# A chunked delta-rule attention on one core: products over the whole TensorE array in place of two 64x64 halves, and the step loop written out

## What is computed

```python
k_n = k / (np.linalg.norm(k, axis=-1, keepdims=True) + 1e-06)
state = np.zeros((B, H, D, D))
for t in range(S):
    y[:, :, t] = q[:, :, t] @ state
    v_old = k_n[:, :, t] @ state
    state = state + beta[:, :, t] * outer(k_n[:, :, t], v - v_old)
...
x = moe(x=y)          # 8 experts, each row goes to one
return moe2(x=x)      # three products, their maximum, one product
```

## Time and profile before

| what | value |
|---|---|
| median of 3 runs | 1251.17 us (1241.86 to 1251.54) |
| profiled execution | 1252.97 us, its span 1251.3 us |
| attention, from 0 to about 550 us | see the rows below |
| routing and sorting | 550 to 605 us |
| first expert layer | 605 to 923 us |
| second expert layer | 923 to 1251 us |
| instructions fetched over the span | 122 packets, 2.00 MB |

### The profile page before, as it was taken

The page is one execution under the profiler, slowest core; times in us unless marked ns, Lnnn a source line. Parts: engine busy times, 40 slices in busy tenths (PEclk is TensorE's granted clock), DMA queues, the critical chain, the costliest instruction groups (busy, mean ns, idle before and its releaser), DMA issues. The chain is left out here.

```text
span 1251.3 us, 38030 instructions
## 1 busy us (share of the span) xinstructions
PE 1025.1 (82%) x16548; PEld 907.0 (72%) x16549; DVE 477.0 (38%) x890; ACT 326.4 (26%) x636; POOL 338.1 (27%) x226
## 2 busy tenths in 40 slices
PE   2688888868868888850598889899959999999999
PEld 2677777767767877740487778787848888888888
DVE  1345454544435454442233343333324232232311
ACT  0334333434323343310121221212212121221211
POOL 3332233223403321118505544415531010000000
PEclk9989998989979899875799999999979999999999
DMA  8501111110111110005323423333320101100000
GB/s 295 217 19 50 36 32 36 48 37 19 50 35 35 33 33 18 3 3 193 119 103 132 138 78 108 127 128 113 113 60 29 32 20 44 31 25 26 1 26 26
DMA packets 34455, 83.51 MB, mean 67 GB/s; under 512 B 4240, under 2 KB 23184, under 8 KB 31760
## 3 DMA queue, kind: packets, MB, share of 16 engines
q1 hardware_dynamic: 28656, 45.22, 11.0%
q0 software_dynamic: 5664, 36.18, 8.7%
HBM read 58.58 MB, written 22.81 MB: 65 GB/s over the span
## 5 line engine op out<-in xcount | busy, mean ns | idle before, releaser
L1011 PE MATMUL hb<-early,last_h 128*128 128x512 f32 x648 | 204.8, 398 | 4.7 <-ACT o_sb L1125 3.6
L1011 PEld LDWEIGHTS hb<-early,last_h 128*128 128x128 f32 x648 | 121.1, 190 | 31.0 <-ACT o_sb L1125 2.7
L1011 PE MATMUL hb<-early,last_l 128*128 128x512 f32 x324 | 127.5, 393 | 0.0
L299 PEld LDWEIGHTS bank<-t,n_hi 64*64 64x64 f16 x2688 | 75.8, 114 | 22.3 <-issue 11.4
L299 PE MATMUL bank<-t,n_hi 64*64 64x64 f16 x2688 | 79.1, 198 | 11.5 <-issue 10.4
L456 ACT CAST t<-bank 128x512 f16<-128x512 f32 x96 | 56.3, 587 | 119.4 <-PE bank L299 117.8
L497 DVE TENSOR_TENSOR p<-bank,cf 128x512 f16<-128x512 f32 x96 | 66.0, 688 | 42.8 <-PE bank L299 41.9
L587 POOL COPY x_all<-y_tile 128x384 f32<-128x384 f32 (+1 forms) x24 | 12.5, 521 | 257.0 <-DVE y_tile L513 257.0
L933 POOL TENSOR_TENSOR late<-w_raw,late 128x3072 fp32r<-128x3072 f32 x8 | 59.7, 7457 | 71.5 <-DVE late L920 71.4
L1149 DVE TENSOR_TENSOR m<-hb,m 128x512 f32<-128x512 f32 x36 | 24.9, 692 | 132.8 <-PE hb L1011 132.8
L1011 PE MATMUL ob<-wo_h,early 128*128 128x384 f32 x288 | 74.2, 335 | 0.0
(11 more groups left out here) (154 smaller groups left out, 2271.6 us busy)
## 6 DMA issues: line engine op xcount, KB each, us to landing
w_raw<-w POOLq DMA_DIRECT2D x14, 1536.0 KB, 7.2
k_raw<-kh SPq DMA_DIRECT2D x24, 256.0 KB, 4.9
kq_t<-qh SPq DMA_DIRECT2D x24, 256.0 KB, 2.8
x_sorted<-zeros SPq DMA_DIRECT2D x32, 192.0 KB, 2.2
x_in<-x_sorted SPq DMA_DIRECT2D x29, 192.0 KB, 2.4
y_sorted<-y_sb SPq DMA_DIRECT2D x28, 192.0 KB, 1.9
v_in<-vh SPq DMA_DIRECT2D x24, 192.0 KB, 2.8
out<-o_sb SPq DMA_DIRECT2D x24, 192.0 KB, 1.9
```

The source lines that it names most:

```text
L299: ins = pe.matmul(out[s, C * u:C * u + C], lhs(s, u), rhs(s, u), start=first and u == 0, stop=True, skip_group_check=True)
L1011: ins = pe.matmul(out, a[x], b[y], start=first and i == 0, stop=last and i == 2, skip_group_check=True)
```

## The change

- **No loops.** `run` writes out all steps on every engine; indices are plain numbers.
- **n_hi block-diagonal.** `n_hi` gets twice the columns, head 0's block and head 1's block on the diagonal and zeros (set once) beside them. The new helper `both_heads` multiplies it in one product over 128 rows and 128 columns in place of two 64x64 ones: in jacobi, prod and resid. `whole` does so for `diagonal`. gram, turn, update, inv and the product with `n_lo` stay as they are.
- **kt from full transposes.** Four 128x128 transposes in place of sixteen 64x64 products.
- **The chain over the whole array.** `state`, `rhs` and `z` get the form [128, pair, 2 heads, 48], zero off the diagonal. "ks" multiplies keys and queries with the state at once (96 columns), "z" is 128 rows to 64 columns, "up" multiplies K' and A with z at once and adds to what "ks" left in the bank. A product of 8 columns precedes it.
- **K' from an own copy of the keys.** Four loads of k for each step rather than two (`k_own`, two buffers), and `kb` is made from it with a factor `beta_k` that DVE works out (NORM part 9).
- **Other engines.** DVE: rhs and the addition to the state in two instructions of 64 partitions each; the copy of y moves to ACT; the reset of the state is a memset at the end of a batch. ACT: n_hi and z in two instructions each, y in one. POOL: n_lo in two. SP: `k_own` loads stand between k and q in the queue, q lands in pieces of 64 numbers.

```diff
-        for w in range(-1, 4):
-            walk_of(w)
-        with eng.Fori(2, STEPS // 2 - 1) as m:
-            body(step(m, 0), step(m - 1, 1), step(m - 1, 0), step(m, 1))
-            body(step(m, 1), step(m, 0), step(m - 1, 1), step(m + 1, 0))
-        for w in range(STEPS - 2, STEPS + 2):
-            walk_of(w)
+        for w in range(-1, STEPS + 2):
+            body(*(k if 0 <= k < STEPS else None for k in (w, w - 1, w - 2, w + 1)))
...
+        def both_heads(lhs, rhs, out, first=False):
+            for u in range(U):
+                ins = pe.matmul(out[:, C * u:C * u + C], lhs[:, u].rearrange("q h c -> q (h c)"), rhs(u), start=first and u == 0,
+                                stop=True, skip_group_check=True)
+            return ins
+        def whole(lhs, rhs, out, first):
+            return pe.matmul(out[:, :], lhs, rhs, start=first, stop=True, skip_group_check=True)
...
-                for u in range(U):
-                    for s in half:
-                        ins = pe.matmul(tb[s, C * u:C * u + C], kn[par][st][s, u, :], ident[s, s], start=u == 0, stop=True,
+                for p in range(NP):
+                    ins = pe.transpose(tb[:, P * p:P * p + P], kn[par][st][:, 2 * p:2 * p + 2, :].rearrange("q h d -> q (h d)"), ident)
...
-                diagonal(ident16, ident_rep, pb, True)
-                each_head(n, eye if lv == 0 else t, pb).then_inc(jacobi_done[st], 1)
+                whole(ident16, ident_rep, pb, True)
+                both_heads(n, lambda u: ident_rep[:, 0:C] if lv == 0 else t16[st][:, u, :], pb).then_inc(jacobi_done[st], 1)
...
-                    for s, r in zip(half, rows):
-                        ins = pe.matmul(out[s, W + D * p:W + D * p + D], kq[r, 0, NP * e + p, :], state[st][r, p, :],
+                    ins = pe.matmul(out[:, W * p:W * p + W], kq_t[par][st][:, NP * e + p, :, :].rearrange("q a t -> q (a t)"),
+                                    state[st][:, p].rearrange("q h d -> q (h d)"), start=p == 0, stop=True, skip_group_check=True)
...
+                pe.matmul(out[0:C, X:X + 8], ident16[:, 0:C], ident16[:, 0:8], start=True, stop=True, skip_group_check=True)
                 for p in range(NP):
-                    for s, r in zip(half, rows):
-                        pe.matmul(out[s, D * p:D * p + D], kq[r, 1, NP * e + p, :], state[st][r, p, :], start=p == 0, stop=False,
...
+                    ins = pe.matmul(out[:, W * p:W * p + W], n_kb_a[par][st][:, NP * e + p, 1:3, :].rearrange("q a t -> q (a t)"),
+                                    z[st][:, p].rearrange("q h d -> q (h d)"), start=False, stop=True, skip_group_check=True)
...
-                act.copy(n_hi[st][:], n_p[par][st][:, :, 0, :]).then_inc(n_hi_ready[st], 1)
+                for hh, s in enumerate(half):
+                    act.copy(n_hi[st][s, :, hh, :], n_kb_a[par][st][s, :, 0, :]).then_inc(n_hi_ready[st], 1)
...
+            elif what == "up":
+                act.wait_ge(up_done[st], 2 * k + e + 1)
+                if e == 0 and k >= 1:
+                    act.wait_ge(x_out[st], k)
+                act.copy(y_tile[st][half[e], :], yb[st][C:P, 0:X]).then_inc(y_out[st], 1)
...
+            for st in range(2):
+                if k >= 2:
+                    sp.wait_ge(kb_ready[st], k - 1)
+                sp.dma_start(k_own[par][st][:], kh[2 * k + st]).then_inc(k_own_in[par], 16)
```

More of the change, by code:

```diff
@@ L39 @@
 CF_BASE = CF_LV + (LEVELS - 2) * C
[L40 to L41 removed]
+CF_TRI = CF_BASE + C
 CF_ONE = CF_TRI + P
@@ L282, in _ @@
             sp.dma_start(raw[:], w[0]).then_inc(arrived, 16)
[L283 to L291, removed]
+        load_k(2, 0)
+        for k in range(2, STEPS):
+            if k + 1 < STEPS:
+                load_k(k + 1, (k + 1) % 2)
+            load_qv(k, k % 2)
     @block.tensor
@@ L313, in eye, with inv @@
             return ident_rep[s, 0:C]
-        def inv(k, m, par, st, what, lv):
+        def inv(k, par, st, what, lv):
             tb, ttb, pb = bank[st]
-            n, nl, t, tt, pr = (lambda s, u, x=x[st]: x[s, u, :] for x in (n_hi, n_lo, t16, tt16, p16))
+            n = n_hi[st]
+            nl, t, tt, pr = (lambda s, u, x=x[st]: x[s, u, :] for x in (n_lo, t16, tt16, p16))
             if what == "kt":
@@ L356, in inv @@
                     pe.sem_inc(passed_pe, 1)
-                each_head(n, t, pb, first=True).then_inc(prod_done[st], 1)
+                both_heads(n, lambda u: t16[st][:, u, :], pb, first=True).then_inc(prod_done[st], 1)
             elif what == "update":
@@ L544, in norm @@
                 dve.wait_ge(s, 6 * k + 6)
-                if not before(k, 1):
+                if k >= 1:
                     for st in range(2):
@@ L548, in norm @@
                 dve.reciprocal(inverse, kept).then_inc(inv_norm, 1)
+            elif part == 9:
+                dve.wait_ge(inv_norm, k + 1)
+                if k >= 2:
+                    for st in range(2):
+                        dve.wait_ge(kb_ready[st], k - 1)
+                own = inverse.rearrange("q (s p h) -> q h s p", s=2, h=2)
+                b = beta[:, 1, 2 * k:2 * k + 2, :].rearrange("q s (p h) -> q h s p", h=2)
+                to = beta_k[par][:].rearrange("q s (e p) -> q e s p", e=2)
+                for e in range(2):
+                    for hh in range(2):
+                        ins = dve.tensor_tensor(to[half[hh], e], own[half[e], hh], b[half[e], hh], ALU.mult)
+                ins.then_inc(beta_k_ready, 1)
@@ L553, in _, with inv @@
+        dve.wait_ge(blank, 1)
         dve.wait_ge(const_in, 64)
-        run(dve, lambda a, c, b, n: walk(a, c, b, n, inv, chain, norm))
+        run(lambda a, c, b, n: walk(a, c, b, n, inv, chain, norm))
     @block.gpsimd
     def _(pool):
-        def inv(k, m, par, st, what, lv):
-            b = beta[:, 2 * k + st, :]
+        latest = [blank, 1]
+        def inv(k, par, st, what, lv):
+            b = beta[:, 0, 2 * k + st, :]
             if what == "kn":
                 pool.wait_ge(inv_norm, k + 1)
-                if not before(k, 2):
+                if k >= 2:
@@ L575, in inv @@
[L575 removed]
+                pool.wait_ge(n_hi_ready[st], 2 * k + 2)
+                pool.wait_ge(*latest)
+                for hh, s in enumerate(half):
+                    if hh == 1:
+                        pool.wait_ge(n_lo_ready[st], 2 * k + 1)
+                    pool.tensor_tensor(n_lo[st][s], n_kb_a[par][st][s, :, 0, :], n_hi[st][s, :, hh, :],
+                                       ALU.subtract).then_inc(n_lo_ready[st], 1)
```

248 lines of the change are left out of this document (121 added, 127 removed).

## The result

The changed kernel took 1206.43 us (median of 4 runs, 1203.6 to 1209.83), the kernel before 1246.86 us in the same job: a ratio of 0.968, 95% interval 0.962 to 0.974. It is faster, by 3.2%, where the forecast said 1.5% of this median (1228). The profiled execution took 1208.53 us with a span of 1206.9, against 1252.97 and 1251.3: 44.4 us less on both counts. All of it lies in the attention: from PE's first record to the first product of the routing it was 533.4 us (20.25 to 553.70) and is 484.4 us (25.07 to 509.45). The start is 4.8 us later, and the time from the routing's first product on is 697.5 us as before.

The account below looks back on a forecast made before the run. PE was taken to bound the attention, not fully: it waited for its own instructions and lost time to the lower clock. The terms summed to -26 us from 1252.97: 1227, rounded 1228 us, range 1188 to 1270.

Parts of the forecast that it names:

- ACT and DVE: Attention: split n_hi and z and the y copy lengthen ACT's work, +13 at n_hi, +8 elsewhere, DVE -1: +20 us.
- kt: kt in the attention: four 128x128 transposes take 0.56 us where 32 records took 0.96: -10 us.
- chain: ks, z and up over the whole array: 2.4 us to an e where it was 2.3: +5 us.
- 16-bit: The 192 groups of 16-bit products over the whole array: eight take about 0.24 us, no gain and no loss: 0.
- forms: PE in the attention: 372 more changes of the product's form at 0.10 us each: +37 us.
- Clock: PE in the attention: fewer idle stretches, so less time at the lower clock: -20 of 32 us.
- Loops gone: Where the attention's loop jumps back: two PE idle times of 6.26 and 6.54 us go: -13 us.
- Fewer instructions: PE's instruction fetch in the attention: 8,592 records for 13,560, stalls shrink to 3 us: -48 us.
- rival D: gram of stream 0 waits 2 us a step because q comes late: 1250 us; chance 0.07.
- A: Rival, PE's array: each change of form costs 0.25 us rather than 0.10, slower at 1284 us; chance 0.13.
- B: Rival: ACT takes PE's place, all its 4.5 us a step show, 1258 us, no change; chance 0.16.
- C: Rival: costs hide, form changes 0.05 us each and the chain at the lower price: 1190 us; chance 0.19.

Follow-up runs that it names:

- e3: The changed kernel with the inverse's products in 64x64 halves again, n_hi and n_lo in one instruction each: 1200.17 us, 0.967 of the kernel before.
- e11: The same kernel as e3, run again: 1200.53 us, 0.963 of the kernel before.
- e4: e1 with n_hi block-diagonal and the waits that needs, without POOL's `passed_pool` increments: 1213.90 us, 0.978 of the kernel before.
- e1: The kernel before with the step loop written out on every engine but SP, nothing else: 1217.57 us, 0.978 of the kernel before.
- e10: e1 without the 14 attention lines where PE raises `passed_pe`, on which nobody waits: 1169.31 us, 0.936 of the kernel before.
- e14: The same kernel as e10, run again: 1167.21 us, 0.934 of the kernel before.
- e9: The changed kernel without the 14 attention lines where PE raises `passed_pe`, on which nobody waits: 1190.91 us, 0.953 of the kernel before.
- e13: The changed kernel with PE's `passed_pe` increments moved behind each group's last product, carrying no wait: 1190.36 us, 0.953 of the kernel before.
- e7: The changed kernel with 432 16-bit products of 8 columns over 128x128 inserted in ks, z and up: 1242.36 us, 1.001 of the kernel before.
- e8: The changed kernel with the insertions of e7 made over 64x64 of the array: 1315.18 us, 1.059 of the kernel before.
- e5: e3 without the 14 attention lines where PE raises `passed_pe`, on which nobody waits: 1179.38 us, 0.950 of the kernel before.
- e2: The changed kernel with 9,936 semaphore increments added to PE's stream: 2617 us, 2.107 of the kernel before.
- e6: The changed kernel with 20 semaphore increments in a row on PE ahead of gram of stream 0, once a step: 1.007 of the kernel before.
- e12: e1 with PE's `passed_pe` increments moved behind each group's last product, carrying no wait: 1199.11 us, 0.960 of the kernel before.

## Why the prediction was right or wrong

The direction was right and the time lies in the range, but the gain is twice what was forecast at its median. For the attention the forecast was -29 us (the sum without the start's +3), measured are -49. PE's time in the attention, sorted by what stands ahead of each idle time of over 0.15 us:

| part of the attention, us | before | changed | difference | forecast |
|---|---|---|---|---|
| the two jumps | 12.8 | 0 | -13 | -13 |
| other stalls ("issue") | 51.7 | 8.1 | -44 | -48 |
| the n_hi place, ACT the last | 6.6 | 17.8 | +11 | +13 |
| waits for DVE and ACT elsewhere | 33.4 | 26.6 | -7 | +7 |
| the rest, PE at work | 429.0 | 431.9 | +3 | +12 (products +32, clock -20) |

- **ACT and DVE, +20. This is the step that failed.** The +13 of the n_hi place, "Elsewhere another 0.6 to 0.7 a step, +8" and DVE's -1 measured +4 together. The n_hi place came out near its price, +11: 0.57 us a step more in stream 0 and 0.24 in stream 1, where the forecast had 1.1 in one. It belongs to the block-diagonal n_hi: 6.5 us in e3 and e11, which make n_hi in one instruction, 15.7 in e4, which has little else of the change. But the waits for DVE and ACT elsewhere did not grow, they shrank by 7 us, and that belongs to the chain's half of the change: they are 33 us in e1, 31 in e4, but 24 in e3 and e11. The forecast had let part of every new ACT instruction show, and had not asked what is covered by the longer groups on PE. That they cover it fits, but no run separates them from the work that moved between DVE and ACT. This term is 16 of the 20 us that the sum missed; the products and the clock are another 9, and the stalls took 4 back.
- **kt -10, chain +5, 16-bit 0, forms +37.** In sum +32; shown by kernels in which the clock hardly falls: PE works 398.8 us in the attention of e10 and e14 and 424.8 in that of e9 and e13, +26. Added up from each group's start-to-start time the changed order comes to 401 us for 368, +33; no run tells where the 7 us between the two lie. The parts: kt's four records 0.49 us (0.56 forecast), `L296` 0.235 us for eight (0.24), a change of form 0.10 (0.10). The chain was too cheap: ks 0.87 to 0.95, z 0.70, up 0.97 and 0.12 for the product ahead of it, 2.7 us to an e for 2.4 before, about +16 us and not +5.
  By the Trainium skill's issue gap ("TensorE: Matmul & The Clock Gate", Back-to-back issue gap) the eight were an estimated 0.20 us; the trace has 0.235, where each product has its own load of 128 columns.
- **Clock, -20.** Right in size: counted only where PE works, the lower level cost at most 27 us before and 6.5 after.
- **Loops gone, -13.** Right for what the jumps show, and blind to what goes with them. Writing the loop out gave 28 us by the ratio (e1): 12 us of other stalls went too, and part of what the clock cost. In the sum that stood under the stalls and the clock.
- **Fewer instructions, -48.** Near in size (-44), wrong in its cause. e10 has the old number of products and 9 us of stalls. The limit that I had read out of the distances (125 records, never under 3.66 us) is there, but what it costs hangs on something that the sum did not have: the increments at the head of each group. With them and the loop written out it costs 40 us (e1), without them 9 to 12.
- **SP and POOL 0, start +3.** No product of `L330` waited for a DMA, so rival D is out. The start was +4.8.
- **Rivals.** A is out by e7 and e8, and the row "0.08 to 0.16" that spoke against it was right. B is out: ACT comes last regularly at the n_hi place alone, 1.09 us in one stream and 0.24 in the other. C said 1190 for cheaper forms and a cheaper chain; a change costs 0.10 as forecast and the chain more, and what came out below the forecast was above all the waits for ACT and DVE.

With the increments gone the new products can be seen by themselves. None of them pays: 0.935 with the old products and the loop written out (e10, e14), 0.950 with the chain and kt over the whole array (e5), 0.953 with all of it (e9). What the loop is worth without the increments no run shows. The first step costs 19 us, the second 4, which is within the intervals; by attention times, 447 (mean of two), 455 and 468 us, the split is the other way round, so only the sum of 22 us is sure. As the change was made, with the increments, its first half is worth 16 us (0.978 to 0.965) and the second none.

What stays open: why increments at the end of a group cost 32 us in the order with 13,560 products and nothing in the one with 8,592, and why the waits for DVE and ACT shrank. 576 instructions more are 2.25 blocks of 256, at 3.7 us an estimated 8 us. The rest would fit an engine that is never far enough ahead to take a late block, but no run shows how far ahead it is.

## What to carry to other kernels

Idle time called "issue" has several owners: a jump, a block of instructions that is late, and a wait that some instruction other than the product carries. Take the carriers away first (put the wait that ends last on the product itself, and drop or move increments that nobody waits for); here that was worth 48 us on the old products and decided whether the new ones pay. Only then is it known whether fewer instructions pay for changes of form at 0.10 us each. A long idle time costs itself and the clock behind it: count both when it goes. And before a new instruction on another engine is priced, look where the bound engine waits for that engine: here it was the n_hi place, and the new ACT work elsewhere did not show.

## What the runs showed of the hardware

- Semaphore increments in PE's own stream: 0.151 us from one to the next in a row, at either level of the clock (e2, e6); 20 in a row are an idle time of 2.2 to 3.9 us (e6).
- A wait that an increment carries: PE starts 0.15 us behind DVE's end, for 0.06 when the product carries it. Where a semaphore instruction of its own carries the wait that ends last, it is 0.14 (e13).
- An idle time of 2 to 4 us: in ten of eleven cases 3.4 or 6.8 us (once 10.2) at the lower clock, from at most 2 us before to 2 us behind its end (e6).
- The instruction queue: one packet of 16 KB to about 250 products and loads (125 records from stall to stall with the increments in front, 124 in e12, up to 127 in e10 without any). Two late ones never lie less than 3.65 us apart but once, 3.38 us (e10).
- The forms 128x128, 128x64 and 64x64 differ for each other alike: 0.10 to 0.11 us for each change, with a 16-bit product of 8 columns in between.
